# Two input tiles change their place in the on-chip memory

## The reference, cut to what matters

```
# x (2, 4096, 192); softmax over the 7 taps of each of 8 heads
w = softmax(weight, axis=-1)                      # (8, 7)
x = sum_k w[h, k] * x_padded[:, s + k, h, :]      # causal window of 7 tokens
h = x @ w_in                                      # 8192 x 192 @ 192 x 2048
P = a0 + a1*h + a2*h**2 + a3*h**3
Q = 1 + |b0|*|h| + |b1|*h**2
x = (P / (Q + 1e-6)) @ w_out                      # back to 192 columns
h = x @ w_in2
out = (s * relu(h)**2 + b) @ w_out2
```

## Time and profile before

| | |
|---|---|
| median of 3 runs | 1280.64 us (1279.2 to 1280.91) |
| the profiled execution | 1280.64 us, its span 1278.8 us |
| TensorE busy | 1258.7 us, 98% |
| VectorE busy | 1131.6 us, 88% |
| ScalarE busy | 1105.5 us, 86% |
| GpSimd busy | 330.5 us, 26% |
| granted TensorE clock, mean | 0.996 |

### The profile page before, as it was taken

One profiled execution on the slowest core, in us unless ns is written; L12 is line 12 of the kernel. 1 busy time (PEld: TensorE's weight loads), 2 busy tenths in 40 slices (PEclk: granted clock), 3 DMA queues, 4 the chain that ended last, 5 costly groups with the idle time before them and its releaser, 6 DMA issues.

```text
span 1278.8 us, 16225 instructions
## 1 busy us (share of the span) xinstructions
PE 1258.7 (98%) x5986; PEld 1070.4 (84%) x5986; DVE 1131.6 (88%) x1047; ACT 1105.5 (86%) x1074; POOL 330.5 (26%) x153
## 2 busy tenths in 40 slices
PE   7999999999999999999999999999999999999999
PEld 4758888888888888888888888888888888888888
DVE  7997899998999989998999989999899998889750
ACT  6898888898898988988898888989889888888853
POOL 3342222322322222222223222222222222232220
PEclk9998999999999999999999999999999999999999
DMA  7100000010000100000000100001000000000000
GB/s 232 49 17 9 1 14 1 1 38 1 12 0 12 25 0 12 0 25 13 0 12 0 37 0 12 0 0 37 0 12 0 12 0 1 13 1 14 1 13 13
DMA packets 14604, 20.39 MB, mean 16 GB/s; under 512 B 1776, under 2 KB 9968, under 8 KB 14320
## 3 DMA queue, kind: packets, MB, share of 16 engines
q1 hardware_dynamic: 14432, 20.01, 5.4%
q10 hardware_dynamic: 144, 0.01, 0.0%
HBM read 13.72 MB, written 6.29 MB: 16 GB/s over the span
## 4 chain that ended last, share of the span: by engine, by line
PE 75%; DVE 13%; issue 6%; POOL 2%; ACT 2%; DMA 1%; SPq 0%; DVEq 0%; ACTq 0%; POOLq 0%
PE o L441 21%; PE o L413 4%; PE h L392 4%; PE h L433 4%; PE h L434 4%; PE h L424 4%; PE h L423 4%; PE h L396 4%; PE o_tail L414 4%; PE h L393 4%; PE h L395 4%; PE h L394 4%; PE h L428 4%; PE o_tail L407 3%; PE o L405 3%
## 5 line engine op out<-in xcount | busy, mean ns | idle before, releaser
L381 POOL TENSOR_TENSOR gl<-work,gh 128x1024 fp32r<-128x1024 f32 x128 | 308.4, 2410 | 848.0 <-ACT gh L642 784.6
L441 PE MATMUL o<-v,work 128*128 128x192 f32 x2048 | 353.3, 326 | 0.0
L441 PEld LDWEIGHTS o<-v,work 128*128 128x128 f32 x2048 | 339.2, 190 | 9.9
L835 DVE SCALAR_TENSOR_TENSOR work<-work,coef,h 128x1024 f32<-128x1024 f32 x128 | 163.7, 1279 | 76.1 <-ACT work L637 73.4
L665 ACT ACTIVATE work<-work 128x1024 f32<-128x1024 f32 x128 | 136.0, 1063 | 58.0 <-DVE work L835 56.5
L636 ACT ACTIVATE work<-h,coef 128x1024 f32<-128x1024 f32 x128 | 154.0, 1203 | 30.8 <-PE h L396 28.2
L873 DVE SCALAR_TENSOR_TENSOR work<-work,coef 128x1024 f32<-128x1024 f32 x128 | 164.5, 1285 | 4.5
L841 DVE SCALAR_TENSOR_TENSOR work<-work,coef,h 128x1024 f32<-128x1024 f32 x128 | 164.0, 1281 | 4.5
L669 ACT ACTIVATE work<-h 128x1024 f32<-128x1024 f32 x128 | 131.2, 1025 | 40.4 <-PE h L434 37.7
L867 DVE SCALAR_TENSOR_TENSOR work<-work,coef 128x1024 f32<-128x1024 f32 x128 | 163.8, 1280 | 0.5
L869 DVE SCALAR_TENSOR_TENSOR work<-work 128x1024 f32<-128x1024 f32 x128 | 159.0, 1242 | 4.4
(11 more groups left out here) (87 smaller groups left out, 2012.1 us busy)
## 6 DMA issues: line engine op xcount, KB each, us to landing
out_dram<-y_out SPq DMA_DIRECT2D x32, 192.0 KB, 2.0
xt<-in_x_main_dram SPq DMA_DIRECT2D x7, 518.0 KB, 5.3
xt_tail<-in_x_tail_dram SPq DMA_DIRECT2D x8, 259.0 KB, 5.5
work<-in_moe_w_out_dram SPq DMA_DIRECT2D x1, 1536.0 KB, 9.3
v<-in_moe_w_out_dram SPq DMA_DIRECT2D x1, 1536.0 KB, 8.3
raw_w_tail_late<-in_moe_w_in_dram SPq DMA_DIRECT2D x4, 256.0 KB, 8.6
work<-in_moe_w_in_dram SPq DMA_DIRECT2D x2, 512.0 KB, 5.6
xt<-in_x_main_dram SPq DMA_DIRECT2D x2, 259.0 KB, 5.3
```

The costliest lines, as they stand in the source:

```text
L381: nc.gpsimd.tensor_tensor(gl[:, j % 2, :], r_buf[j % 2], gh[:, j % 2, :].bitcast(F32), ALU.subtract).then_inc(gl_ready, 1)
L441: return pe.matmul(o2[:, c // 2, c % 2, 0:D], g, v2[:, f, :], start=(f == 0 and c % 2 == 0), stop=(f == FT - 1), skip_group_check=True)
L835: nc.vector.scalar_tensor_tensor(q_buf[buf], w_of_n, b0_abs, h_flat, ALU.add, ALU.mult).then_inc(z_done, 1)
```

## The change

Two lines move up in the list of tiles: `xt` and `xt_tail` are asked for ahead of `conv` instead of behind `bias_row`. Nothing else is edited.

```
         tail_diag = [work2[:, 2, k * P:(k + 1) * P] for k in range(TAPS)]
 
+        xt = sb("xt", [P, 2, HALO + TOK])
+        xt_tail = sb("xt_tail", [P, HALO + TOK])
         conv = sb("conv", [P, 2, TOK])
         conv_tail = sb("conv_tail", [P, TOK])
         x1_hi = [sb(f"x1_hi{i}", [P, TOK], F32R) for i in range(2)]
...
         bias_row = sb("bias_row", [P, D])
-        xt = sb("xt", [P, 2, HALO + TOK])
-        xt_tail = sb("xt_tail", [P, HALO + TOK])
         cw = sb("cw", [P, 2, TAPS])
```

## The result

The changed kernel takes 1292.83 us in the median (1292.51 to 1293.81), the one before 1280.91 on the same chip: a ratio of 1.0095, interval 1.0083 to 1.0106. It is 12 us slower. The forecast was no change, 1278.6 to 1282.7 us, with 0.10 on slower. It was wrong.

The account below looks back on a forecast made before the run. The prediction took TensorE's pace between product starts as the bound, its terms making 1237.1 of 1278.8 us. The change's five parts were each 0, leaving 1280.64 us, range 1278.6 to 1282.7.

Parts of the forecast that it names:

- What bounds the kernel: TensorE's steady part, 160 to 1270 us: the distance between product starts sets the time, 0.227 us per wide product.
- The 14 ns beside the columns: TensorE's wide fp32r products: 0.227 us between starts, against 0.2133 us for 512 columns at 2.4 GHz.
- the moving operand's remainder: 2560 wide TensorE products reading moved tiles: starting at 32 instead of 0 modulo 64 bytes adds 0 ns per product.
- the region: Where in memory TensorE's moved tiles lie: the move up by 6240 bytes was taken to cost 0.
- The upper bound of +18.2 us: 2560 wide products on moved tiles: one more 64-byte piece per 2048-byte row, 7.1 ns each.
- the first rival: Wide TensorE products on moved tiles slow by 3.5 to 7 ns each, giving 1289.6 to 1298.8 us; chance 0.06.
- The half-clock row: TensorE from 27.03 to 28.31 us: wide products start 0.427 us apart, exactly 512 columns at 1.2 GHz.
- The second rival: TensorE's weight loads: 27 waits for GpSimd's subtraction lose 0.12 us each, 3.3 us in all, giving 1277.3 us; chance 0.03.
- VectorE, ScalarE, stationary loads of the taps and the stores at 0: Work on moved tiles outside the moving operand: 0 each; ends -1.0 to +1.0 us for VectorE, 0 to +0.2 for stores.
- The half-clock stretches: TensorE near 23.6 to 27.0 and 97.2 to 104.3 us: keep their places; rival shift to 1283.9 or 1277.3 us, chance 0.05.
- The range: Whole kernel: 1278.6 to 1282.7 us, from run-to-run spread of 1.7 us and small ends of VectorE and the stores.
- The test named at the end: TensorE product groups: L392 to L396 lengthening while L405 and L406 don't would show wide products on moved tiles slowed.

Follow-up runs that it names:

- the last experiment: A kernel of TensorE products alone, not an edit of either kernel: moving tile 0 to 256 bytes off the weights, several data types; float32 took 6.87 us from group to group throughout.

## Why the prediction was wrong

- *What bounds the kernel* was right: the pace between starts on TensorE, and nothing else in the steady part. The 14 ns beside the columns were seen and left unexplained.
- *The failed step is the moving operand's remainder, "I take 0 ns per product".* In the undisturbed units of the traces it was 6.6 ns for each product on a moved tile, 131 ns per unit, and 40 ns more on those behind them. The row it went by was of another kind: the taps are plain float32, and the last experiment shows that float32 stays at 0.429 us from 0 to 256 bytes. A row of the same line shape was taken for a row of the same resource. The trace had no fp32r product off its place, which the text said; the value should then have stood nearer the middle of its bounds, and the chance of slower well above 0.10.
- *The question was also put wrongly.* It asked about the region and the remainder modulo 64 of the moved tile by itself. The runs show that the partner is the weight slice, which didn't move, and the period 256 bytes.
- *The upper bound of +18.2 us*, and with it the first rival (3.5 to 7 ns, 1289.6 to 1298.8 us), held the measured 1292.8, but partly by luck. Its 7.1 ns were one more 64-byte piece per row; the runs show no such piece, since a shift of all tiles by 32 bytes costs nothing. And the 12 us are about 21 from the slower pace, the tail on `gh` and `gl` included, less what the waits gave back, which the rival's price didn't have.
- *The half-clock row* was used against the rival: no read limit at 1.2 GHz. It was right as read (0.427 us after the change too), but says nothing of 2.4 GHz, where the kernel spends its time.
- *The second rival* had GpSimd's waits as a gain in case of fewer collisions. They did shrink, and 8 us came back, but as what a slower TensorE no longer needs to wait for; without that the loss would be about 20 us. The prediction wanted the weight load's waits near 14 us in sum, and they are 6.6.
- *VectorE, ScalarE, stationary loads of the taps and the stores at 0*: right. L849 has a median of 611 ns where it had 610, and the run with those tiles off has 0.9998. The half-clock stretches kept their places: clock 0.996 in both executions.
- *The range* doesn't follow from the ends that were named for it: 1280.6 with 1.7 us of spread and 1.0 of VectorE on both sides, and 0.2 of the stores, is 1277.9 to 1283.5 and not 1278.6 to 1282.7. The result lies outside both.
- *The test named at the end* ("L392 to L396 lengthen while L405 and L406 don't") fired only by half: L405 stayed, but L406 went from 391 to 397 ns with the others. A slowed product spoils those that follow.

The Trainium skill, "SBUF — State Buffer", Who interferes with whom, gives TensorE two independent read ports, one for the moving operand and one for the weight load. For fp32r with 512 columns at the full clock the runs disagree: the pace depends on where the two reads stand to each other, 0.227 to 0.234 us. The same section says that TensorE never waits on anyone; of other engines that agrees with the runs, as the slowing came with all of them idle (0.232 us per step at the program's end). The 16-byte lines of the page's Specifications, which the prediction weighed, don't decide it either, since 32 bytes are two whole lines and cost 6 ns.

That the two reads collide in banks of the memory is an inference that no run here tests. What is shown is the distance, its period, the data type, the clock, and that no other engine is needed. Why 64 bytes are cheaper than 32 or 96, why products of 256 columns don't care, and what makes the tail short or long stays open.

## What to carry to other kernels

A change of allocation order is a change of time where TensorE runs fp32r products back to back: keep the moving tiles and the weights at the same remainder modulo 256 bytes, and round odd-sized tiles (here 4144 and 2072 bytes) up to a multiple of 256 or put them last. A cheap test for it is one pad of 32 bytes in front of the moving tiles. In a forecast, a neighbouring row stands in for a missing one only if data type and clock are the same.

## What the runs showed of the hardware

- fp32r, 512 columns, 2.4 GHz: 0.227 us per product at distance 0 modulo 256 bytes, 0.229 at 64, 0.233 to 0.234 at 32, 96, 128, 160, 192 and 224; 0.427 at 1.2 GHz with the x tiles 0 or 96 bytes off.
- Starts 4 to 16 bytes on take 0.231 to 0.238 us (most at 4), even if both operands are shifted alike.
- What counts is the weight slice that is loaded beside the product. A badly placed product also slows between one and ten well placed ones behind it.
- float32 (0.429 us per recorded instruction) and bf16 (0.216 us) with 512 columns, and fp32r with 256 columns (0.118 to 0.120 us), show no dependence from 0 to 256 bytes; bf16 is faster than fp32r at its best by 11 ns per product.
